# Expert attention with the turned probabilities as the moving operand, and two score passes on stacked queries, in a retention + MLP + expert-attention kernel

## The chip, the cores and the metric

The kernel runs as one program on one core of a Trainium2 chip. The metric is the device time in microseconds (us). The kernel before the change takes 551.65 us, the median of 3 runs (549.74 to 553.75). All durations below come from one profiled execution of it.

The core's engines work side by side and wait for each other through semaphores: TensorE (PE in the rows; PEld is its weight load), VectorE (DVE), ScalarE (ACT), GpSimd (POOL), and SyncE (SP), which here only issues DMAs.

## The reference, cut to what matters

```python
# 1. retention over q, k, v of (2, 8, 768, 64)           -> x (2, 768, 512)
# 2. x = x + relu(layernorm(x) @ w_ch1) @ w_ch2            (512 -> 2048 -> 512)
# 3. top-2 of 4 experts, each a causal attention of its own:
logits = x @ w_gate                          # (2, 768, 4)
w = softmax over the two largest logits
for e in range(4):
    q, k, v = x @ wq[e], x @ wk[e], x @ wv[e]          # (2, 768, 64) each
    scores = q @ k.T / 8, causal
    a = exp(scores - rowmax); a /= a.sum(-1) + 1e-9    # (2, 768, 768)
    ye = a @ v @ wo[e]                                 # (2, 768, 512)
    out += (w of this expert where it is chosen) * ye
```

All of it is float32. The change is in part 3 alone.

## The kernel before, in words

Every float32 product on TensorE is made of rounded parts: an operand is split into a high part (`hi`, rounded to the matmul format) and the rest (`lo`). ScalarE writes `hi` out of PSUM, VectorE subtracts and writes `lo`, and TensorE makes three passes, hi·hi, hi·lo and lo·hi (`PASSES`). Queries are tiled by 128 rows, six tiles for each of the two batches.

The program is an order written out by hand for each engine; semaphores only say when a step may start. Part 3 works on *units*: one unit is a query tile `i` of a batch `b` against its (i+1)·128 keys. `TILES = (5, 0, 4, 1, 3, 2)` puts a long and a short one together, so each *pair* of units has 7·128 = 896 score columns. One expert is 6 pairs, four experts are 24 pairs. A pair goes through these steps:

- `scores`: TensorE, 3 passes of q (stationary) against k (moving, up to 512 columns). q and k of the two batches lie on 64 rows each; the other batch's rows of k are zeros. A bf16 matmul adds the causal mask (`masked`).
- `row_max` on VectorE, `exponent` on ScalarE (exp with the sum of the row, `den`), `sum_plus`/`sum_inverse` on VectorE, `z_factor` on GpSimd (expert weight over the sum, one number a row).
- `turn_a`: TensorE transposes the 7 blocks of the pair into PSUM; `a_t_hi` (ScalarE) and `a_t_lo` (VectorE) write the two parts of the turned probabilities.
- `attend`: for each key block, `a_t` hi and lo are stationary and the 128 columns of `ev` (64 of v hi, 64 of v lo) are moved past them: 14 matmuls of 128 columns a pair.
- `z_lows` (ScalarE) and `z_add` (VectorE) scale and add the two halves of the result.

In four of the six pairs (`FILL`) TensorE also makes a quarter of the next expert's q and k (`expert_qk`, 12 matmuls of 384 columns), which `project_out` takes out of PSUM on ScalarE, `keys_lo` on VectorE and `queries_hi`/`queries_lo` per tile on both. In the last expert, `turn_z`, `z_t_hi`, `z_t_lo`, `output` and `output_out` follow each pair. Experts 0 to 2 are a hardware loop (`Fori`) on most engines, so each turn of it also spends register instructions on the counts to wait for.

In a pair, TensorE's order is `turn_a`, `scores` of the pair one ahead, `expert_qk`, `attend`.

Of the kernel before, what the change touches and what calls it, by code (L numbers as in the profile page):

```python
# [32 lines left out]
P = 128  # L33
# [36 lines left out]
def retention_moe_program(nc, q, k, v, g_ln, w_ch1, w_ch2, w_gate, wq, wk, wv, wo, out):  # L70
# [5 lines left out]
    NC = S // P  # L76
    KT = DM // P
# [5 lines left out]
    G = 3  # L83
    VG = E * D + E
# [12 lines left out]
    with ExitStack() as ctx:  # L97
# [6 lines left out]

        x = sb(ctx, "x", [P, NIT, NC, P])
# [19 lines left out]
        x2, w_o, eq_t = {}, {}, {}  # L125
# [46 lines left out]
        neg_max = sb(ctx, "neg_max", [P, 2])  # L172
        den = sb(ctx, "den", [P, B * NC])
        inv_den = sb(ctx, "inv_den", [P, B * NC])
        z_scale = sb(ctx, "z_scale", [P, B * NC])
        z_low = sb(ctx, "z_low", [P, 2, D])
        a = sb(ctx, "a", [P, 2, S])
        a_t = {part: sb(ctx, f"a_t_{part}", [P, 2, NC, P], F32R) for part in ("hi", "lo")}
        z = sb(ctx, "z", [P, B * NC, E * D])
        out_sb = sb(ctx, "out_sb", [P, 3, DM])  # L180
# [34 lines left out]
        s_pj, s_eqn, s_ekhi, s_eklo = (sem(n) for n in ("s_pj", "s_eqn", "s_ekhi", "s_eklo"))  # L215
        s_eqhi, s_eqlo, s_zero = sem("s_eqhi"), sem("s_eqlo"), sem("s_zero")
        s_sc, s_max, s_exp = sem("s_sc"), sem("s_max"), sem("s_exp")
        s_at, s_athi, s_atlo = sem("s_at"), sem("s_athi"), sem("s_atlo")
        s_pv, s_den, s_scl, s_zlow, s_z = (sem(n) for n in ("s_pv", "s_den", "s_scl", "s_zlow", "s_z"))
        s_wohi, s_wo, s_zt, s_zthi, s_ztlo = (sem(n) for n in ("s_wohi", "s_wo", "s_zt", "s_zthi", "s_ztlo"))  # L220
        s_out, s_osb = sem("s_out"), sem("s_osb")
# [35 lines left out]
        UNITS = [(TILES[2 * m_ + w], b) for m_ in range(3) for b in range(B) for w in range(2)]  # L257
        LAST_USE = {i: max(u for u, (i_, b) in enumerate(UNITS) if i_ == i) for i in TILES}
        NU = len(UNITS)
        PAIRS = NU // 2  # L260
        PJ = [(b, h) for b in range(B) for h in range(2)]
        HALF = S // 2


# [6 lines left out]
        def v_bank(t):  # L271


            return ps[:, t % 2 if t < EARLY else (6, 7, 3, 6)[t - EARLY], 0:VG]

        def ahead(e, p_):

            return (e, p_) if p_ < PAIRS else (e + 1, p_ - PAIRS)

# [3 lines left out]
        def sc_bank(u, a0, a1):  # L283

            return (flat(2, 3, a1) if u % 2 else flat(0, 2, a1))[:, a0:a1]

        def pj_bank(e, n):

            return ps[:, 2 + n if isinstance(e, int) and e == 0 else 3, 0:HALF]

        def at_bank(u, n):
            return flat(7, 8, n) if u % 2 else flat(4, 6, n)


# [1074 lines left out]
```

## Time and profile before

| | us |
|---|---|
| median of 3 runs | 551.65 |
| the profiled execution, its own time | 551.49 |
| its span, first to last instruction | 549.7 |
| TensorE busy | 526.0 (96%) |
| VectorE busy | 214.0 (39%) |
| ScalarE busy | 183.0 (33%) |
| GpSimd busy | 85.9 (16%) |
| granted clock, mean | 0.994 of full speed |
| retention | 0 to about 97 |
| MLP | about 97 to 374 |
| values, gate, q and k of expert 0 | 374 to 404 |
| four experts' attention | 404 to 549.7 |

The span is what lies between the first and last instruction; 1.8 us of the execution's time lie around it. The duration of a matmul in a row includes its pipeline, so neighbours overlap: how fast TensorE works is read from how far apart the starts lie, and the chain of waits gives a run of matmuls its length in that sense (12 matmuls of 512 columns in 2.80 us).

### The profile page before, as it was taken

How to read it: one execution, taken by the hardware profiler on the slowest of the kernel's cores; microseconds unless marked ns; L12 is line 12 of the kernel's file. 1: busy time of each engine (PE TensorE's matmuls, PEld its weight loads, DVE VectorE, ACT ScalarE, POOL GpSimd, SP SyncE). 2: the span in 40 equal slices, each digit the busy share in tenths (PEclk: the TensorE clock that was granted, in tenths of full speed). 3: DMA queues.
4: the chain of work that ended last, by engine and by line, in shares of the span. 5: the costliest groups of instructions: out<-in, count | busy, mean ns of one | idle time of the engine just before them, and what ended most of it. 6: DMA issues, size and time to landing. Idle time of an engine off the chain costs nothing.

```text
span 549.7 us, 8473 instructions
## 1 busy us (share of the span) xinstructions
PE 526.0 (96%) x3064; PEld 458.1 (83%) x3064; DVE 214.0 (39%) x519; ACT 183.0 (33%) x451; POOL 85.9 (16%) x113
## 2 busy tenths in 40 slices
PE   3999897999999999999999999999999999999997
PEld 2989897888888888888888888889989898988885
DVE  2444546313221422211141111235366565656562
ACT  3334341211010220101031101224466757667553
POOL 3000010899970000000000000005010100100000
PEclk9999998899999999999999999999999999999999
DMA  9474660344440000000000000000000000000123
GB/s 189 72 149 89 129 150 20 97 135 135 134 116 0 1 0 0 0 0 0 0 0 0 1 0 1 0 2 20 1 20 1 21 0 0 0 0 0 39 77 116
DMA packets 57948, 23.56 MB, mean 43 GB/s; under 512 B 45760, under 2 KB 54080, under 8 KB 57920
## 3 DMA queue, kind: packets, MB, share of 16 engines
q1 hardware_dynamic: 57920, 23.18, 17.7%
q8 instruction: 18, 0.29, 0.2%
q14 instruction: 10, 0.08, 0.0%
HBM read 20.03 MB, written 3.15 MB: 42 GB/s over the span
## 4 chain that ended last, share of the span: by engine, by line
PE 83%; DVE 7%; issue 5%; ACT 3%; POOL 1%; DVEq 0%; ACTq 0%; POOLq 0%
PE ps L567 24%; PE ps L576 24%; PE ps L667 5%; PE ps L711 4%; PE ps L684 4%; PE ps L487 3%; PE ps L643 3%; PE ps L734 3%; PE ps L508 3%; PE ps L696 2%; PE ps L500 2%; PE ps L513 2%; PE ps L475 2%; DVE neg_max L1263 1%; DVE scaled_k L252 1%
## 5 line engine op out<-in xcount | busy, mean ns | idle before, releaser
L1157 DVE SCALAR_TENSOR_TENSOR h_t_lo<-ps,h_t_hi 128x512 fp32r<-128x512 f32 x48 | 33.2, 691 | 200.0 <-ACT h_t_hi L843 200.0
L843 ACT ACTIVATE h_t_hi<-ps 128x512 fp32r<-128x512 f32 x48 | 28.7, 599 | 221.8 <-PE ps L567 221.8
L567 PE MATMUL ps<-xn_t_hi,w_hi 128*128 128x512 f32 x192 | 76.3, 397 | 0.9 <-DVE xn_t_lo L1152 0.9
L576 PE MATMUL ps<-w_hi,h_t_hi 128*128 128x512 f32 x192 | 76.1, 396 | 0.0
L567 PE MATMUL ps<-xn_t_lo,w_hi 128*128 128x512 f32 x192 | 75.9, 395 | 0.0
L567 PE MATMUL ps<-xn_t_hi,w_lo 128*128 128x512 f32 x192 | 75.7, 394 | 0.0
L576 PE MATMUL ps<-w_hi,h_t_lo 128*128 128x512 f32 x192 | 75.5, 393 | 0.0
L576 PE MATMUL ps<-w_lo,h_t_hi 128*128 128x512 f32 x192 | 74.6, 389 | 0.0
L567 PEld LDWEIGHTS ps<-xn_t_hi,w_hi 128*128 128x128 f32 x192 | 36.1, 188 | 9.3 <-issue 1.1
L567 PEld LDWEIGHTS ps<-xn_t_hi,w_lo 128*128 128x128 f32 x192 | 36.2, 189 | 8.6
L567 PEld LDWEIGHTS ps<-xn_t_lo,w_hi 128*128 128x128 f32 x192 | 36.3, 189 | 8.2
L576 PEld LDWEIGHTS ps<-w_hi,h_t_lo 128*128 128x128 f32 x192 | 36.0, 188 | 8.4
L576 PEld LDWEIGHTS ps<-w_lo,h_t_hi 128*128 128x128 f32 x192 | 36.1, 188 | 8.0
L576 PEld LDWEIGHTS ps<-w_hi,h_t_hi 128*128 128x128 f32 x192 | 36.0, 188 | 7.5
L937 ACT ACTIVATE a<-ps,neg_max 128x768 f32<-128x768 f32 (+5 forms) x48 | 30.0, 631 | 36.8 <-DVE neg_max L1263 36.8
L433 POOL TENSOR_TENSOR w_qk_lo<-raw_qk,w_qk_hi 128x512 fp32r<-128x512 f32 x4 | 5.1, 1280 | 229.3 <-ACT w_qk_hi L895 229.3
L711 PE MATMUL ps<-ev,a_t_hi 128*128 (+1 forms) x168 | 38.4, 272 | 0.7 <-DVE z_t_lo L1294 0.5
L711 PE MATMUL ps<-ev,a_t_lo 128*128 (+1 forms) x168 | 38.8, 275 | 0.0
L711 PEld LDWEIGHTS ps<-ev,a_t_hi 128*128 128x128 f32 x168 | 32.2, 191 | 1.9 <-DVE a_t_lo L1269 1.2
L1269 DVE TENSOR_TENSOR a_t_lo<-ps,a_t_hi 128x512 fp32r<-128x512 f32 (+2 forms) x64 | 30.1, 494 | 5.8 <-ACT a_t_hi L943 5.7
L711 PEld LDWEIGHTS ps<-ev,a_t_lo 128*128 128x128 f32 x168 | 32.2, 192 | 0.1
L487 PE MATMUL ps<-q_t,k_t 128*128 128x128 f32 x192 | 27.4, 289 | 1.6 <-ACT q_t L793 1.6
(136 smaller groups left out, 966.2 us busy)
## 6 DMA issues: line engine op xcount, KB each, us to landing
raw_w<-in_moe_w_ch SPq DMA_DIRECT2D x32, 256.0 KB, 2.6
raw_k<-in_k SPq DMA_DIRECT2D x16, 192.0 KB, 3.8
raw_q<-in_q SPq DMA_DIRECT2D x16, 192.0 KB, 4.3
raw_v<-in_v SPq DMA_DIRECT2D x16, 192.0 KB, 3.2
out_y<-out_sb SPq DMA_DIRECT2D x12, 256.0 KB, 2.0
raw_vg<-in_moe_wv SPq DMA_DIRECT2D x4, 128.0 KB, 2.9
raw_wo<-in_moe_wo SPq DMA_DIRECT2D x1, 512.0 KB, 4.7
raw_qk<-in_moe_wq SPq DMA_DIRECT2D x4, 128.0 KB, 2.1
```

The costliest lines, as they stand in the source:

```text
L487: mm = pe.matmul(s_bank(it, m_)[:, c, j], k_t[:, it % 2, 2 * m_ + c, j, :], q_t[:, it % 2, 2 * m_ + c, :], start=True, stop=True)
L508: mm = pe.matmul(y_bank(it, m_)[:, c % 2, j], prob[:, m_, c % 2, j, :], raw["v"][:, it % 2, c, j], start=(j == 0), stop=(c == 0), skip_gro ...
L567: mm = pe.matmul(ps[:, f % 2, :], w1[a_][:, f, kk, :], xn_t[b_][:, kk, :], start=(kk == 0 and p_ == 0), stop=(kk == KT - 1 and p_ == 2))
L576: mm = pe.matmul(ps[:, 2 + tau, :], h_t[a_][:, f % 2, tau * P:(tau + 1) * P], w2[b_][:, f, :], start=(f == 0 and p_ == 0), stop=(f == NF - ...
L643: mm = pe.matmul(v_bank(t), x2[a_][:, b, kk, c * P:(c + 1) * P], w_vg[b_][:, kk, :], start=(kk == 0 and p_ == 0), stop=(kk == KT - 1 and p ...
L667: mm = pe.matmul(pj_bank(e, n), w_qk[a_][:, kk, :], x2[b_][:, b, kk, half * HALF:(half + 1) * HALF], start=(kk == 0 and p_ == 0), stop=(kk ...
L684: mm = pe.matmul(sc_bank(u, a0, a1), eq_t[a_][:, i * P:(i + 1) * P], ek_t[b_][:, e % 2, b, a0:a1], start=(p_ == 0), stop=(p_ == 2 and not ...
L711: mm = pe.matmul(z_bank(u), a_t[a_][:, u % 2, sc, :], ev[:, b * NC + sc, e], start=(sc == 0 and a_ == "hi"), stop=(sc == i and a_ == "lo"))
L843: act.activation(h_t["hi"][:, f % 2, :], ps[:, f % 2, :], ACT.Relu).then_inc(s_hhi, 1)
L937: act.activation(a[:, u % 2, 0:n], sc_bank(u, 0, n), ACT.Exp, bias=neg_max[:, u % 2:u % 2 + 1], accum_out=den[:, u:u + 1]).then_inc(s_exp, 1)
L1157: dve.scalar_tensor_tensor(h_t["lo"][:, f % 2, :], ps[:, f % 2, :], 0.0, f32(h_t["hi"][:, f % 2, :]), ALU.max, ALU.subtract).then_inc(s_hl ...
L1269: dve.tensor_tensor(a_t["lo"][:, u % 2].rearrange("p c t -> p (c t)")[:, a0:a1], at_bank(u, a1)[:, a0:a1], f32(a_t["hi"][:, u % 2].rearran ...
```

## The change: what it does

1. **Attend.** The operands change sides: `ev` of a key block (128 columns: v hi and v lo) is stationary, and the turned probabilities are moved past it, three query tiles at a time (up to 384 columns, fewer at the diagonal). For that, `a_t` of three tiles is kept side by side (`a_top` for tiles 0 to 2, `a_low` for 3 to 5), and `attend(h)` runs once per *half* (expert and batch: 3 pairs), not once per pair: 18 matmuls for three pairs where there were 42. Units are now ordered by batch.
2. **z.** Its result comes out already turned, 128 rows by 384 columns, so `turn_z` and `z_t` from PSUM go. `z_lows`, `z_add` handle 64×384 tiles; new steps `z_round` (ScalarE) and `z_rest` (GpSimd) split z into hi and lo.
3. **Scaling.** A factor per row can no longer be applied after `attend`, so GpSimd's `weigh` multiplies the whole probabilities (896 columns a pair) before they are turned. Scores are now made two pairs ahead.
4. **Scores.** `q_both` holds q hi on rows 0 to 63 and q lo on rows 64 to 127; `k_twice` holds the same k on both. Two passes (k hi, k lo) give all four products. The second copy of k is a DMA from rows 64–127 to rows 0–63 (`repeat_k`, 8 an expert).
5. **Projection.** `project_lo` on VectorE now makes both k lo and q lo, 64×384 each; `queries_hi`/`queries_lo` and the zeroing of `ek_t` go.
6. **Start and end.** All `values` and the gate come before `expert_qk(0, ...)`; the hardware loops become plain repeated code; the outputs of batch 0 are made in the last two pairs, those of batch 1 after the last `attend`.

```diff
-        UNITS = [(TILES[2 * m_ + w], b) for m_ in range(3) for b in range(B) for w in range(2)]
+        UNITS = [(i, b) for b in range(B) for i in TILES]
-        FILL = (0, 1, 2, 4)
+        FILL = {1: 0, 2: 1, 4: 2, 5: 3}
...
+            def repeat_k(e, n):
+                b, half = PJ[n]
+                cols = slice(half * HALF, (half + 1) * HALF)
+                for part, s in (("hi", s_ekhi), ("lo", s_eklo)):
+                    sp.wait_ge(s, len(PJ) * e + n + 1)
+                    sp.dma_start(f32(k_twice[part][0:D, e % 2, b, cols]),
+                                 f32(k_twice[part][D:2 * D, e % 2, b, cols])).then_inc(s_twice[b], 16)
...
+            def weigh(g, w):
+                e, b, i, u, c0, c1 = span_of(g, w)
+                if w == 0:
+                    pool.wait_ge(s_den, 2 * g + 2)
...
+                pool.tensor_scalar(a[:, g % 2, c0:c1], a[:, g % 2, c0:c1], inv_den[:, u:u + 1],
+                                   weight[:, u, e:e + 1], ALU.mult, ALU.mult).then_inc(s_weighed, 1)
...
-                    for p_, (a_, b_) in enumerate(PASSES):
-                        mm = pe.matmul(sc_bank(u, a0, a1), eq_t[a_][:, i * P:(i + 1) * P],
-                                       ek_t[b_][:, e % 2, b, a0:a1], start=(p_ == 0), stop=(p_ == 2 and not diagonal))
+                        for part in ("hi", "lo"):
+                            mm = pe.matmul(sc_bank(g, a1)[:, a0:a1], q_both[:, e % 2, b, i * P:(i + 1) * P],
+                                           k_twice[part][:, e % 2, b, a0 - c0:a1 - c0],
+                                           start=(part == "hi"), stop=(part == "lo" and not diagonal))
...
-                for sc in range(i + 1):
-                    for a_ in ("hi", "lo"):
-                        mm = pe.matmul(z_bank(u), a_t[a_][:, u % 2, sc, :], ev[:, b * NC + sc, e],
-                                       start=(sc == 0 and a_ == "hi"), stop=(sc == i and a_ == "lo"))
+            def attend(h):
+                e, b = divmod(h, B)
+                for low in range(2):
+                    pe.wait_ge(s_atlo, at_count(G * (h + 1)))
+                    if h >= 1:
+                        pe.wait_ge(s_zsum, 2 * h - 1 + low)
+                    for s in (s_eqlo, s_eklo):
+                        pe.wait_ge(s, pieces_before(G * (h + 1)))
+                    last = G * (low + 1) - 1
+                    for sc in range(last + 1):
+                        skip = max(0, sc - G * low) * P
+                        for part in ("hi", "lo"):
+                            mm = pe.matmul(z_bank(low == 0)[:, skip:HALF],
+                                           ev[:, b * NC + sc, e].rearrange("p h d -> p (h d)"),
+                                           (a_low if low else a_top)[part][:, sc, skip:HALF], ...)
...
+            def slot(g):                                   # TensorE
+                e, p_ = divmod(g, PAIRS)
+                if g + 2 < LAST:
+                    scores(g + 2)
...
+                if g % G == 0 and g > 0:
+                    attend(g // G - 1)
+                turn_a(g)
+                if e < E - 1 and p_ in FILL:
+                    expert_qk(e + 1, FILL[p_], g)
...
+            def slot(g):                                   # VectorE
...
+                if g % G == 0:
+                    if g + 2 < LAST:
+                        for w in range(2):
+                            row_max(g + 2, w)
+                        sums(g + 2)
+                    if g > 0:
+                        for top in range(2):
+                            z_add(2 * (g // G) - 2 + top)
+                    for w in range(2):
+                        a_t_lo(g, w)
+                else:
+                    for w in range(2):
+                        if g + 2 < LAST:
+                            row_max(g + 2, w)
+                        a_t_lo(g, w)
+                    if g + 2 < LAST:
+                        sums(g + 2)
+                if e < E - 1 and p_ in FILL:
+                    project_lo(e + 1, FILL[p_])
```

How the order moves on VectorE, in a pair of the expert loop that has a fill piece. Names: `a_t_lo` and, in the change, `a_low_lo`, `a_top_lo` are the turned probabilities' low parts, `neg_max` the row maxima, `inv_den` the row sums, `ek_t_lo`/`k_twice_lo` the keys' low part. Before:

```order
L1278 TENSOR_SCALAR inv_den<-den 128x2 [waits s_exp]
L1268 REGISTER_ALU
L1269 TENSOR_TENSOR a_t_lo<-ps,a_t_hi 128x512 [waits s_athi]
L1268 REGISTER_ALU
L1269 TENSOR_TENSOR a_t_lo<-ps,a_t_hi 128x128 [waits s_athi]
L1282 ISA
L1283 RECIPROCAL inv_den<-inv_den 128x2 [waits s_den]
```

and with the change, the second pair of a half:

```order
L1290 TENSOR_REDUCE neg_max<-ps 128x1 [waits s_sc]
L1299 TENSOR_TENSOR a_low_lo<-ps,a_low_hi 128x4x128 [waits s_athi]
L1290 TENSOR_REDUCE neg_max<-ps 128x1 [waits s_sc]
L1299 TENSOR_TENSOR a_low_lo<-ps,a_low_hi 128x128 [waits s_athi]
L1299 TENSOR_TENSOR a_top_lo<-ps,a_top_hi 128x2x128
L1309 TENSOR_SCALAR inv_den<-den 128x2 [waits s_weighed,s_exp]
L1311 RECIPROCAL inv_den<-inv_den 128x2 [waits s_den]
L1280 TENSOR_TENSOR k_twice_lo<-ps,k_twice_hi 64x384 [waits s_ekhi]
L1283 SCALAR_TENSOR_TENSOR q_both<-ps,q_both 64x384 [waits s_eqhi]
```

The maxima now stand between the low parts, and the low part of q has joined that of k; register instructions are gone.

On ScalarE the same pair reads as follows with the change (`a,den<-ps,neg_max` is `exponent`, `k_twice_hi` and `q_both` are `project_out`):

```order
L975 ACTIVATE a_low_hi<-ps 128x4x128
L964 ACTIVATE a,den<-ps,neg_max 128x768
L975 ACTIVATE a_low_hi<-ps 128x128
L975 ACTIVATE a_top_hi<-ps 128x2x128
L964 ACTIVATE a,den<-ps,neg_max 128x128
L953 ACTIVATE k_twice_hi<-ps 64x384
L955 ACTIVATE q_both<-ps 64x384
```

The first `exponent` now stands between the two parts of `a_t_hi`; before, all of `a_t_hi` came first, in one run, and the exponents after it.

On TensorE, at the boundary between two halves (`k_twice` against `q_both` is `scores`, `a_top_hi,ev` is `attend`):

```order
L713 MATMUL ps<-x_hi,w_qk_lo 128x384
L731 MATMUL ps<-k_twice_hi,q_both 128x512 [waits s_exp,s_twice0,s_eqlo]
L731 MATMUL ps<-k_twice_lo,q_both 128x512
L735 MATMUL ps<-masked,ident_bf 128x128
L731 MATMUL ps<-k_twice_hi,q_both 128x384
L731 MATMUL ps<-k_twice_lo,q_both 128x384
L735 MATMUL ps<-masked,ident_bf 128x128
L762 MATMUL ps<-a_top_hi,ev 128x384 [waits s_eqlo,s_eklo,s_zsum,s_atlo]
```

`attend` waits for the low parts of the projection of the pair just before it (`s_eqlo`, `s_eklo`), since its PSUM banks are those that the projection used.

## Rows read from the trace of the kernel before

**Rows 1.** Page, the granted clock in 40 slices of the span, in tenths.
```profile
PEclk9999998899999999999999999999999999999999
```

**Rows 2.** Busy time by stretch (one expert): stretch, length, each engine's busy us (instructions), clock.
```profile
470.50:503.00 32.50, 32.34 (x234) 30.03 (x234) 20.33 (x62) 21.52 (x67) 1.16 (x6) 1.00 0.00 0
```

**Rows 3.** Chain of waits, one pair of expert 1: start us, us, what.
```profile
442.39 1.51 PE ps L711 x14
443.90 0.79 PE ps L696 x7
444.69 0.97 PE ps L684 x6
...
445.74 0.40 PE ps L684 x3
446.21 2.16 PE ps L667 x12
```

**Rows 4.** Chain of waits: values, projection of expert 0, gate's end, last expert, last eviction.
```profile
383.68 4.35 PE ps L643 x36
388.03 8.45 PE ps L667 x48
...
407.30 0.05 DVE weight L1243
...
519.95 1.42 PE ps L734 x6
...
522.13 0.44 PE ps L721 x4
...
546.66 0.60 ACT out_sb L965
```

**Rows 5.** Timeline, ScalarE and VectorE in that pair: start, us, instruction, [idle before <-releaser].
```profile
440.31 0.15 DVE L1283 RECIPROCAL inv_den<-inv_den 128x2 f32<-128x2 f32 x1
440.38 0.27 DVE L1269 TENSOR_TENSOR a_t_lo<-ps,a_t_hi 128x128 fp32r<-128x128 f32 x1
440.57 1.14 DVE L1263 TENSOR_REDUCE neg_max<-ps 128x1 f32<-128x768 f32 x2
441.55 0.90 ACT L937 ACTIVATE a<-ps,neg_max 128x768 f32<-128x768 f32 x1 [1.31 <-DVE neg_max L1263]
442.44 0.36 ACT L937 ACTIVATE a<-ps,neg_max 128x128 f32<-128x128 f32 x1
443.28 0.49 ACT L919 ACTIVATE ek_t_hi<-ps 64x384 f32 x1
443.99 0.56 DVE L1251 TENSOR_TENSOR ek_t_lo<-ps,ek_t_hi 64x384 f32 x1 [1.47 <-ACT ek_t_hi L919]
444.03 0.52 ACT L950 ACTIVATE z_low<-ps,z_scale 128x64 f32<-128x64 f32 x2 [0.26 <-PE ps L711]
444.44 1.04 ACT L943 ACTIVATE a_t_hi<-ps 128x512 fp32r<-128x512 f32 x3
```

**Rows 6.** Groups by line and shape, from 385 us on, VectorE and GpSimd.
```profile
L1269 DVE TENSOR_TENSOR a_t_lo<-ps,a_t_hi 128x512 fp32r<-128x512 f32 x24 | 16.5, 686 | 5.8 <-ACT a_t_hi L943 5.7
L1269 DVE TENSOR_TENSOR a_t_lo<-ps,a_t_hi 128x256 fp32r<-128x256 f32 x16 | 6.5, 408 | 0.0
L433 POOL TENSOR_TENSOR w_qk_lo<-raw_qk,w_qk_hi 128x512 fp32r<-128x512 f32 x3 | 3.8, 1281 | 14.3 <-ACT w_qk_hi L895 14.3
```

**Rows 7.** Groups by line and shape, whole span, GpSimd.
```profile
L409 POOL TENSOR_SCALAR w_hi<-raw_w 128x512 fp32r<-128x512 f32 x16 | 10.0, 623 | 74.2 <-DMA raw_w<-in_moe_w_ch 74.2
```

**Rows 8.** Page, a DMA: engine, count, KB each, median us from issue to landing.
```profile
raw_qk<-in_moe_wq SPq DMA_DIRECT2D x4, 128.0 KB, 2.1
```

**Rows 9.** Timeline of TensorE at the end of retention.
```profile
93.73 0.77 PE L500 MATMUL ps<-raw_v,scaled_k 128*128 128x128 f32 x2 [1.58 <-DVE state L1043]
```

**Rows 10.** Busy time by stretch, columns as in rows 2: the clock around it.
```profile
92.00:93.00 1.00, 0.15 (x2) 0.00 (x0) 0.96 (x4) 0.00 (x0) 0.00 (x0) 0.88 0.00 0
...
99.00:100.00 1.00, 1.00 (x7) 0.86 (x6) 0.00 (x0) 0.71 (x2) 1.00 (x2) 0.71 0.00 0
```

More of the change, by code:

```diff
@@ L102, in sem @@
             return ctx.enter_context(nc.semaphore(name))
+        with ExitStack() as late:
+            z_t = {part: sb(late, f"z_t_{part}", [P, 2, B, S], F32R) for part in ("hi", "lo")}
         x = sb(ctx, "x", [P, NIT, NC, P])
@@ L116, in retention_moe_program @@
             state = sb(early, "state", [P, NC - 1, P])
+        with ExitStack() as late:
+            z_low = sb(late, "z_low", [P, 2, HALF])
+            z_sum = sb(late, "z_sum", [P, 2, HALF])
         raw_vg = sb(ctx, "raw_vg", [P, KT, VG])
@@ L316, in norm_groups, with pj_bank, pieces_before, out_bank @@
+        FILL = {1: 0, 2: 1, 4: 2, 5: 3}
+        def pj_bank(n):
+            return ps[:, 6 + n % 2, 0:HALF]
+        def pieces_before(g):
+            return len(PJ) + sum(1 for g_ in range(g) if g_ < LAST - PAIRS and g_ % PAIRS in FILL)
+        def out_bank(o):
+            return ps[:, o % 2, :]
         def norm_groups(n):
@@ L462, in _ @@
+            for q in range(2 * HALVES - 2, 2 * HALVES):
+                z_rest(q)
         @block.tensor
@@ new lines, in expert_qk @@
+                if len(PJ) * e + n >= 2:
+                    pe.wait_ge(s_eqlo, len(PJ) * e + n - 1)
+                    pe.wait_ge(s_eklo, len(PJ) * e + n - 1)
+                if g >= G:
+                    pe.wait_ge(s_zsum, 2 * (g // G))
+                for kk in range(KT):
+                    for p_, (a_, b_) in enumerate(PASSES):
+                        mm = pe.matmul(pj_bank(n), w_qk[a_][:, kk, :], x2[b_][:, b, kk, half * HALF:(half + 1) * HALF],
+                                       start=(kk == 0 and p_ == 0), stop=(kk == KT - 1 and p_ == 2))
@@ new lines, in a_t_lo, with sums @@
+            def a_t_lo(g, bank):
+                dve.wait_ge(s_athi, at_count(g) + 1 if bank == 0 else at_count(g + 1))
+                for part in at_parts(g):
+                    if part[0] == bank:
+                        dve.tensor_tensor(a_t("lo", part), at_source(g, part), f32(a_t("hi", part)),
+                                          ALU.subtract).then_inc(s_atlo, 1)
+            def sums(g):
+                u = span_of(g, 0)[3]
+                pair = slice(u, u + 2)
+                dve.wait_ge(s_exp, 2 * g + 2)
+                if g >= PAIRS:
+                    dve.wait_ge(s_weighed, 2 * (g - PAIRS) + 2)
@@ L1346, in _ @@
             gate_out()
-            with dve.Fori(0, E - 1) as e:
-                expert(e, False)
-            expert(E - 1, True)
-            z_t_lo(PAIRS - 1)
+            for n in range(3):
+                project_lo(0, n)
+            for w in range(2):
+                row_max(0, w)
+            sums(0)
+            project_lo(0, 3)
+            for w in range(2):
+                row_max(1, w)
+            sums(1)
+            for g in range(LAST):
+                slot(g)
+            for q in range(2 * HALVES - 2, 2 * HALVES):
+                z_add(q)
+            for o in range(NC + 1, 2 * NC, 2):
+                output_out(o)
 _INS = ["q", "k", "v", "moe_g_ln", "moe_w_ch1", "moe_w_ch2", "moe2_w_gate", "moe2_wq", "moe2_wk", "moe2_wv", "moe2_wo"]
```

549 lines of the change are left out of this document (250 added, 299 removed).

## The prediction, made before the changed kernel ran

> **What bounds the kernel now.** I read the clock first: it is full nearly everywhere, also in all of the attention stage [rows 1]. Then the busy time by stretch. One expert takes 32.5 us, and in it TensorE is busy for 32.34, ScalarE 21.5, VectorE 20.3, GpSimd 1.2 [rows 2]. Then the chain of waits inside a pair: it runs through TensorE alone, 1.51 attend, 0.79 transposes, 0.97 + 0.40 scores (the masks add 0.07 each), 2.16 projection, together 5.97 us [rows 3]. So in the middle of an expert TensorE sets the pace. But the timeline of the same pair shows how near the next bound is: ScalarE waits only 0.26 us for `attend` before `z_low` [rows 5]. ScalarE and VectorE hand work to each other and back, in strict order, and that ring is nearly as long as TensorE's list. That is the point on which this prediction turns.
>
> **TensorE: what goes.** Attend: 14 matmuls of 128 columns in 1.51 us is 0.108 each [rows 3], 336 of them 36.2 us. By widths, 384 columns take 0.18 (12 in 2.16 [rows 3]), 260 take 0.121 (36 in 4.35 [rows 4]), 128 take 0.108. A half now has ten of 384, four of 256, four of 128: 1.80 + 0.48 + 0.43 = 2.7 us, eight halves 21.7. Saved: 14.5. Scores: the third of three passes, (0.97 + 0.40)/3 = 0.46 a pair, 24 pairs: 11.0. `turn_z`: 0.44 a pair, six: 2.6 [rows 4]. Together 28 us less TensorE work. A half (three pairs) then needs scores 3 × 1.05, transposes 3 × 0.79, projection 2 × 2.16, attend 2.7: 12.6 us, where it took 16.3.
>
> **The ring of ScalarE and VectorE: what stays.** I walk VectorE's list for one half, since it is the engine that is waited for. On VectorE the next instruction starts 0.08 before the last one's end (0.27 at 440.38, next at 440.57 [rows 5]), so I take duration less 0.08; on ScalarE three `a_t_hi` take 1.04, so the second part costs 0.55 after the first. Handing over costs about 0.04: the first maximum took 0.94 and the exponent began 0.98 after it began [rows 5]. In the first three experts register instructions still lie in such gaps; the change has none.
>
> - Second pair: max 768 0.87; `a_t_lo` 512 0.61 [rows 6]; max 128 0.28 (with its end, as the exponent needs both); 0.04; exponent 768 0.89 to the next start [rows 5]; `a_t_hi` 128+256 0.55, which stands behind that exponent in ScalarE's queue; 0.05; `a_t_lo` 128+256 0.19+0.33 [rows 5, 6]; the two small sum operations 0.30 (0.15 each [rows 5], one waits for the other); k lo and q lo 0.48 each (0.56 [rows 5]; the second operation I take like the first). Sum 5.1.
> - Third pair: the same with 640/256 and 384 in place of 768/128 and 128+256: 4.9 (the long max and exponent are 0.1 shorter each).
> - First pair: maxima 1.15, both exponents 1.35 with the last one's accumulator, sums 0.30, two `z_add` of 64×384 0.96, `a_t_lo` 1.13, hand-overs and short waits for `z_low` and `a_t_hi` 0.3. Sum 5.2.
>
> A half is 15.2. TensorE's part in it: `attend` can't start before the last q lo, as its banks are the projection's, and `z_low` of its second part and the transposes behind it then arrive 0.1 late. So 15.3 us a half, where TensorE needs 12.6 and stands still for 2.7, in one piece, ahead of `attend`. Check of the method on before: the ring of a pair with projection gives 5.4 to 5.7 against TensorE's 5.97, and the 0.26 wait agrees. So each half gains 1.0 us, not 3.7: the rest of the saving becomes a wait.
>
> GpSimd hides: `weigh` of 896 columns costs 1.1 to 1.3 by 0.62 for 512 [rows 7], `z_rest` 1.0 by 1.28 for 512 [rows 6]; 7 us of `weigh` an expert beside 30.6, and scores are two pairs ahead, so nobody waits. If that cover went, each pair would pay 1.3. The DMA copies of k (about 2.1 us to land [rows 8]) are needed more than 3 us after they are issued, except at the start.
>
> **The start.** Values now end at 388.03 + 4 × 1.45 = 393.8 [rows 4]. The gate's chain ends 3.9 later: in before the last values ended at about 388.03 + 8.45 projection + 5.8 values + 1.5 scores of a pair = 403.8 and the gate at 407.35 [rows 3, 4], 3.6 later, and I add 0.3, since no other work lies between the gate's steps now. From there, one behind the other: k lo and q lo of two pieces (to +6.0), the copy of k (+7.8), scores (+8.9), maxima and exponents of the first pair (+11.6), fourth projection piece on both engines (+13.1), the same for the second pair (+15.9). So the first pair's ring begins at 409.7, some 5 us later than in before. What was filled with values before is a wait now.
>
> **Sum.** 409.7, first half without z 14.2, then 423.9; five halves of 15.3: 500.4; one half without projection, 15.3 − 1.9 = 13.4: 513.8. End: z of the last but one half is split 5.95 later, then TensorE is dense: six outputs of 1.42 [rows 4] and two transposes, 10.2, `attend` 2.7; the turned z goes through four engines' steps (0.5 + 0.5 + 0.5 + 1.0, the first part hidden behind `attend`'s second), 1.1 more; six outputs 8.6; eviction and last DMA 3.2 (549.7 − 546.66 in before [rows 4], and 0.2 for the pipeline's end). That is 31.8 and an end at 545.6. Around the span lie 1.8 us: 547.4.
>
> **The clock.** At the end of retention TensorE stood still for 1.58 us after sparse work [rows 9], and the clock fell to half, from within the slice at 92 until within the slice at 99 [rows 10]. The change adds a stand-still of 2.7 us in each half. Work around it is denser than it was there, so I don't expect a fall each time. What one costs: while the clock is at 1.2 GHz, `attend` and the transposes behind it, 3.5 us, take up to twice as long, and in the first pair of a half VectorE waits for them. I price a fall at 1.7 (partly beside `attend`) to 3.0 (all of `attend` and some transposes) and put two of them at 1.7 into the number: 547.4 + 3.4 = **551 us**, against the profiled 551.5 and the median 551.65. No change that can be measured: I take 1%, 5.5 us, as what a measurement tells.
>
> The Trainium skill (TensorE: Matmul & The Clock Gate, "Why this matters for your kernels") advises against idle gaps of TensorE of a length that a gap of 2.7 us does not reach. By that rule no fall would come, and the time would be 547.4; the trace before speaks against it, with a fall after 1.58 us.
>
> **Rivals.**
>
> A. *Slower: the clock falls in nearly each half.* Seven stand-stills at 3.0 each are 21: 547.4 + 21 = 568. It decides from 9.5 us of falls in all on (above 557), three to five of them. For it: the fall in rows 9 and 10 after a shorter stop, and that the stop sits right ahead of the work on which VectorE waits. Against: the full clock through retention [rows 1], where TensorE also waits in each iteration, though shorter. Chance 0.22.
>
> B. *The ring is shorter than I walk it.* If ScalarE and VectorE overlap more (no register instructions, hand-overs of nearly nothing), a half might be 14.3; 6.9 halves give 7 less and fewer stops: 541. Against: each term is a measured duration. Chance 0.15.
>
> C. *TensorE keeps the pace, as the change hopes.* Then 551.5 − 28 + 5 at the start = 528. It needs VectorE's list to run without the waits for ScalarE (1.5 us in each pair, as the 1.47 in rows 5), which the order forbids. Chance 0.07.
>
> D. *My forecast*: the ring sets the pace, with none to three falls, 547 to 556. Chance 0.56.
>
> **Numbers.** Faster by over 1% (below 546.1): B, C and a little of D, 0.26. Slower by over 1% (above 557.2): A and a little of D, 0.24. Within: 0.50. The range leaves out C and the worst of A: 539 to 565. Unknown in D itself: the start (±2) and 0.2 in each pair's ring (±4).
>
> **What would show it.** In the profile after: an expert of 30 to 31 us; VectorE and ScalarE each busy for 20 to 21 of it; the chain of waits in the loop going through VectorE and ScalarE and not TensorE; TensorE waiting before `attend` for `q_both` of the piece before; the second part of `a_t_lo` waiting for ScalarE in each pair. Attend's matmuls at 0.18 apart and 144 of them; score matmuls 128. The clock below full in some stretches behind those waits would show the price of the stop. Wrong would be: TensorE without waits in the loop (then C), or waits on GpSimd's `a` or on the copies of k, which I hold for hidden.

## The result: 580.2 us, 5% slower, and outside the range

The changed kernel takes 580.2 us (median of 4 runs, 579.5 to 581.1) against 552.0 (549.7 to 553.8) for the kernel before on the same chip: ratio 1.051 [1.047, 1.056]. Forecast were 551, with a range to 565. The profiled execution has a span of 577.7 us, where the sum without clock falls gave 545.6.

First the page of the changed kernel: the granted clock, and the copies of k.

```profile
PEclk9999997999999999999999999999798779997789
k_twice_hi<-k_twice_hi SPq DMA_DIRECT2D x16, 96.0 KB, 2.1
```

Where [rows 1] show a full clock, there are now gaps from slice 29 on (each is 14.4 us; slice 29 begins at 404 us). The copies land in 2.1 us, as assumed, and in the loop no engine's list of waits names them.

Then the busy time by stretch, columns as in [rows 2]: stretch, length, busy us (instructions) of TensorE, its weight load, VectorE, ScalarE and GpSimd, then the clock, the DMA share and GB/s. A stretch is one half (three pairs), cut where VectorE starts the two maxima of the half's first pair. The first half has no `attend`, five have everything, the seventh has no projection, and the last stretch is the last half with the end.

```profile
405.00:421.25 16.25, 11.49 (x60) 10.55 (x59) 10.21 (x25) 9.12 (x25) 6.69 (x9) 0.79 0.12 29
421.25:439.80 18.55, 12.81 (x85) 11.79 (x85) 11.11 (x26) 11.10 (x29) 6.27 (x9) 1.00 0.09 22
439.80:461.58 21.78, 17.00 (x85) 16.04 (x85) 11.11 (x26) 10.70 (x28) 7.54 (x10) 0.76 0.13 31
461.58:482.52 20.94, 15.92 (x85) 14.90 (x85) 11.12 (x26) 11.34 (x29) 6.27 (x9) 0.84 0.08 19
482.52:501.28 18.76, 12.82 (x85) 11.80 (x85) 11.13 (x26) 10.71 (x28) 7.53 (x10) 1.00 0.09 22
501.28:521.56 20.28, 14.37 (x85) 13.36 (x85) 11.11 (x26) 10.59 (x28) 6.29 (x9) 0.92 0.08 21
521.56:539.59 18.03, 13.03 (x62) 11.52 (x63) 8.69 (x22) 8.75 (x24) 5.06 (x7) 0.72 0.04 10
539.59:577.70 38.11, 28.41 (x129) 24.02 (x129) 11.34 (x23) 11.86 (x26) 6.84 (x8) 0.87 0.22 83
```

Two things are to be read here. In the two halves at full clock TensorE is busy for 12.8 us, as the 12.6 of the forecast, so its work did go down. But those halves take 18.55 and 18.76 us, 18.65 on average, where 15.3 were forecast, and no engine is busy for more than 13 of them. The five halves that have everything take 20.06 us on average; what is over 18.65 goes with the clock, which is below full in the other three.

What fills the 18.55 is in the timeline of the first such half (TensorE, ScalarE, VectorE; most rows left out).

```profile
421.25 1.16 DVE L1290 TENSOR_REDUCE neg_max<-ps 128x1 f32<-128x512 f32 x2
421.32 0.41 PE L762 MATMUL ps<-a_top_hi,ev 128*128 128x384 f32 x1 [2.09 <-DVE q_both L1283]
...
424.01 0.95 PE L746 MATMUL ps<-ident,a 128*128 128x128 f32 x7
...
425.06 0.69 ACT L964 ACTIVATE a<-ps,neg_max 128x512 f32<-128x512 f32 x1 [4.51 <-PE ps L746]
...
426.44 0.17 DVE L1309 TENSOR_SCALAR inv_den<-den 128x2 f32<-128x2 f32 x1 [4.03 <-ACT a L964]
...
428.79 1.05 PE L746 MATMUL ps<-ident,a 128*128 128x128 f32 x7 [2.75 <-DVE a_low_lo L1299]
...
429.09 0.95 DVE L1290 TENSOR_REDUCE neg_max<-ps 128x1 f32<-128x768 f32 x1
...
432.47 0.29 DVE L1299 TENSOR_TENSOR a_low_lo<-ps,a_low_hi 128x128 fp32r<-128x128 f32 x1 [1.50 <-ACT a_top_hi L975]
...
434.57 0.82 DVE L1290 TENSOR_REDUCE neg_max<-ps 128x1 f32<-128x640 f32 x1
...
437.66 0.56 DVE L1299 TENSOR_TENSOR a_top_lo<-ps,a_top_hi 128x384 fp32r<-128x384 f32 x1 [1.33 <-ACT a_top_hi L975]
...
439.80 1.16 DVE L1290 TENSOR_REDUCE neg_max<-ps 128x1 f32<-128x512 f32 x2
```

`L1290` are the maxima, `L762` is `attend`, `L746` the transposes (`turn_a`), `L964` the exponents, `L1309` the first of the two sum steps, `L1299` the low parts. The maxima are ready 1.2 us after 421.25, but the exponents start at 425.06, behind the transposes (L746). `exponent(g + 2)` writes the buffer `a[:, g % 2]` that `turn_a(g)` reads, and so waits for `s_at` (lines 961 to 963); and in the first pair of a half `turn_a(g)` stands on TensorE behind the 2.7 us of `attend`, which itself waits for VectorE's last `q_both`. So the ring, in which VectorE and ScalarE hand work to each other, is closed by a detour over TensorE. VectorE stands still for 4.0 us, and TensorE stands still twice: 2.09 ahead of `attend`, 2.75 ahead of the transposes of the second pair. The list of waits of the changed kernel sums it up (who <- for whom: us, times, longest):

```profile
DVE inv_den L1309 <- ACT a L964: 40.8, 10, 5.7
ACT a L964 <- PE ps L746: 38.5, 7, 6.2
...
PE ps L746 <- DVE a_low_lo L1299: 19.3, 7, 2.8
...
PE ps L762 <- DVE q_both L1283: 15.8, 6, 3.2
```

The forecast had also named waits on GpSimd's `a` as a sign of being wrong. The list has one, TensorE's weight load for the transposes, 17.2 us in 6 times. But GpSimd had finished the product of that pair at 421.46 (the last one begins at 420.90 and takes 0.56), 7 us before these transposes start; the low parts named above are what they waited for last. In the loop GpSimd is hidden, as forecast.

The second loss is the clock. In the timeline of TensorE, the two stops of the next half:

```profile
440.03 0.41 PE L762 MATMUL ps<-a_top_hi,ev 128*128 128x384 f32 x1 [3.15 <-DVE q_both L1283]
449.05 1.73 PE L746 MATMUL ps<-ident,a 128*128 128x128 f32 x7 [2.75 <-DVE a_low_lo L1299]
```

And the busy time of three stretches around them, columns as above:

```profile
442.00:444.00 2.00, 2.00 (x10) 2.00 (x9) 0.00 (x0) 0.00 (x0) 0.00 (x0) 0.50 0.57 130
...
446.00:448.00 2.00, 0.30 (x4) 0.17 (x2) 1.12 (x4) 1.95 (x7) 0.82 (x2) 1.00 0.00 0
...
450.00:452.00 2.00, 2.00 (x9) 2.00 (x8) 1.19 (x3) 0.87 (x2) 1.22 (x2) 0.50 0.00 0
```

At each of the two stops the clock goes to 0.50, that is 1.2 GHz. The first fall comes after the stop, when `attend` has run for about 1.2 us (1.00 until 441.20, 0.61 from there to 441.60, then 0.50); the second comes within the stop (1.00 until 448.00, 0.50 from 448.30 on). `attend`, for which both other engines wait, takes 4.1 us from its first start to its last end, where it took 2.9 in the half before.

### The profile page after: what moved, and what is told of

Its sections match the earlier page's. It is cut to its first block, busy times and chain, and to the rows that moved or that the text cites. A ratio compares the mean times of both kernels' runs of the same rounds, so it can differ in the third digit from the quotient of the medians.

```text
span 577.7 us, 7555 instructions
## 1 busy us (share of the span) xinstructions
PE 509.9 (88%) x2784; PEld 447.6 (77%) x2784; DVE 218.8 (38%) x475; ACT 178.5 (31%) x403; POOL 126.3 (22%) x151
## 3 DMA queue, kind: packets, MB, share of 16 engines
HBM read 20.03 MB, written 3.15 MB: 40 GB/s over the span
## 4 chain that ended last, share of the span: by engine, by line
PE 76%; DVE 11%; ACT 6%; issue 5%; POOL 1%; ACTq 0%; DVEq 0%; POOLq 0%
PE ps L610 23%; PE ps L619 23%; PE ps L762 5%; PE ps L530 3%; PE ps L780 3%; PE ps L713 3%; PE ps L686 3%; PE ps L746 3%; PE ps L551 2%; ACT a L964 2%; DVE a_low_lo L1299 2%; PE ps L543 2%; DVE neg_max L1290 2%; PE ps L556 2%; PE ps L518 2%
## 5 line engine op out<-in xcount | busy, mean ns | idle before, releaser
L610 PE MATMUL ps<-xn_t_hi,w_hi 128*128 128x512 f32 x192 | 74.9, 390 | 0.8 <-DVE xn_t_lo L1182 0.8
L610 PE MATMUL ps<-xn_t_lo,w_hi 128*128 128x512 f32 x192 | 74.7, 389 | 0.0
L473 POOL TENSOR_SCALAR a<-a,inv_den,weight 128x768 f32<-128x768 f32 (+5 forms) x48 | 34.0, 719 | 117.6 <-DVE inv_den L1311 117.6
L964 ACT ACTIVATE a<-ps,neg_max 128x768 f32<-128x768 f32 (+5 forms) x48 | 30.4, 634 | 61.7 <-PE ps L746 38.5
L746 PE MATMUL ps<-ident,a 128*128 128x128 f32 x168 | 28.3, 317 | 19.7 <-DVE a_low_lo L1299 19.3
L746 PEld LDWEIGHTS ps<-ident,a 128*128 128x128 f32 x168 | 22.3, 165 | 21.8 <-POOL a L473 17.2
L1290 DVE TENSOR_REDUCE neg_max<-ps 128x1 f32<-128x768 f32 (+5 forms) x48 | 28.8, 617 | 0.5
L1299 DVE TENSOR_TENSOR a_low_lo<-ps,a_low_hi 128x512 fp32r<-128x512 f32 (+2 forms) x40 | 21.4, 554 | 18.0 <-ACT a_top_hi L975 10.5
```

The costliest lines, as they stand in the source:

```text
L473: pool.tensor_scalar(a[:, g % 2, c0:c1], a[:, g % 2, c0:c1], inv_den[:, u:u + 1], weight[:, u, e:e + 1], ALU.mult, ALU.mult).then_inc(s_we ...
L610: mm = pe.matmul(ps[:, f % 2, :], w1[a_][:, f, kk, :], xn_t[b_][:, kk, :], start=(kk == 0 and p_ == 0), stop=(kk == KT - 1 and p_ == 2))
L746: mm = pe.transpose(flat(4, 6, s0 + P)[:, s0:s0 + P], a[:, g % 2, s0:s0 + P], ident[:, :])
L964: act.activation(a[:, g % 2, c0:c1], sc_bank(g, c1)[:, c0:c1], ACT.Exp, bias=neg_max[:, 2 * (g % 2) + w:2 * (g % 2) + w + 1], accum_out=de ...
L1290: top = dve.tensor_reduce(neg_max[:, 2 * (g % 2) + w:2 * (g % 2) + w + 1], sc_bank(g, c1)[:, c0:c1], AX.X, ALU.max, negate=True)
L1299: dve.tensor_tensor(a_t("lo", part), at_source(g, part), f32(a_t("hi", part)), ALU.subtract).then_inc(s_atlo, 1)
```

## The experiments

All times are medians, ratios against the kernel before of the same session (551.0, 551.6, 552.0 and 552.3 us).

**The transposes ahead of attend.** On TensorE, in the first pair of a half:

```diff
+                turn_a(g)
                 if g % G == 0 and g > 0:
                     attend(g // G - 1)
-                turn_a(g)
```

> The changed kernel, with turn_a ahead of attend in the first pair of each half on TensorE (two lines swapped), nothing else. Theory 1, the missed wait: exponent of the pair two ahead overwrites the buffer that turn_a reads, so it waits for turn_a, and turn_a stands behind attend; VectorE then sits for 5.7 us in each half. Swapped, the exponents run beside attend, and a half at full clock goes from 18.6 to about 16.3 us: seven halves give 14 to 17 less, 563 to 566 us, and VectorE's 5.7 us waits for the exponents go. Theory 2, the clock: the halves are long because TensorE runs at 1.2 GHz in them; the swap only moves where it stands still, and the time stays within 5 us of 580.

Measured: 556.9 us, ratio 1.010 [1.006, 1.013]: 23 less, more than expected. Its first half at full clock and its first half below it:

```profile
421.88:437.82 15.94, 13.03 (x85) 11.70 (x85) 11.12 (x26) 11.12 (x29) 6.25 (x9) 1.00 0.11 26
437.82:455.50 17.68, 14.62 (x85) 13.30 (x85) 11.21 (x26) 10.68 (x28) 7.50 (x10) 0.90 0.16 38
```

A stretch of 2 us inside the second:

```profile
440.00:442.00 2.00, 2.00 (x9) 2.00 (x8) 0.89 (x3) 0.84 (x3) 1.14 (x2) 0.50 0.58 131
```

Its group of the first step of the row sums, which waits for both exponents (busy us, mean ns | idle before it, releaser):

```profile
L1309 DVE TENSOR_SCALAR inv_den<-den 128x2 f32<-128x2 f32 x24 | 4.1, 169 | 14.1 <-ACT a L964 14.1
```

In its first half at full clock, that step of the sums and the first maximum of the second pair:

```profile
424.44 0.17 DVE L1309 TENSOR_SCALAR inv_den<-den 128x2 f32<-128x2 f32 x1 [1.41 <-ACT a L964]
...
427.11 0.95 DVE L1290 TENSOR_REDUCE neg_max<-ps 128x1 f32<-128x768 f32 x1
```

A half at full clock takes 15.94 for 18.55, and VectorE waits 1.41 us for 4.03: the missed wait cost 2.6 us a half. What VectorE waits for exponents falls from 40.8 to 14.1 us. The clock still falls, in three of the five halves, which take 17.5 to 17.7.

**Other work in the stops.** Small bf16 matmuls, whose result nobody reads, in the two stops, 18 and 24 of them:

```diff
+            def keep_busy(g, n):
+                pe.wait_ge(s_exp, 2 * g + 4)
+                for _ in range(n):
+                    pe.matmul(sc_bank(g + 1, P)[:, :], ident_bf[:, :], masked[:, :], start=True, stop=True,
...
+                if g % G == 0 and G <= g < LAST - G:
+                    keep_busy(g, 18)
+                if g % G == 1 and G < g < LAST - G:
+                    keep_busy(g, 24)
```

> The changed kernel with filler matmuls (bf16, 128 columns, into a score bank that is free then) in TensorE's two stops of a half: 18 ahead of attend, 24 ahead of the transposes of the second pair. They take 1 to 2.7 us of stops of 2 to 4 us and compute nothing that is used. Theory 1 (missed wait): only what the half clock costs goes, 20.1 to 18.6 us a half, six halves and less at the end: 568 to 572 us. Theory 2 (clock first): the granted clock of the attention stage goes from about 0.85 to nearly 1, and with it the time from 580 to about 557, since 47 us at 1.2 GHz cost up to 23.

Measured: 574.4 us, ratio 1.040 [1.033, 1.048]: 6 less. That is above theory 1's 572, with single executions from 570.3 to 577.9, and far from theory 2's 557. Two of its halves:

```profile
442.03:460.75 18.72, 15.48 (x127) 14.11 (x127) 11.11 (x27) 10.58 (x28) 7.54 (x10) 1.00 0.15 36
460.75:481.07 20.32, 17.07 (x127) 15.71 (x127) 11.13 (x27) 11.23 (x29) 6.27 (x9) 0.92 0.09 21
```

Four of the five halves now run at full clock and take 18.5 to 18.8; the fifth is the second row. This parts the two losses: five times (20.06 - 18.65) is 7 us of clock, and 18.65 instead of 15.3 has nothing to do with it.

**The order in ScalarE's and VectorE's lists.** In the second and third pair both parts of `a_t_hi` ahead of both exponents, and both maxima ahead of both low parts (ScalarE's side; VectorE's is alike):

```diff
                     for w in range(2):
                         a_t_hi(g, w)
-                        if g + 2 < LAST:
+                    if g + 2 < LAST:
+                        for w in range(2):
                             exponent(g + 2, w)
```

> The changed kernel with ScalarE's order in the second and third pair of a half made a_t_hi, a_t_hi, exponent, exponent, and VectorE's row_max, row_max, a_t_lo, a_t_lo. Nothing is removed. If the ring of ScalarE and VectorE is what sets these pairs (as the prediction had it), VectorE no longer waits 1.3 to 1.5 us for the part behind the exponent, a pair with projection goes from 5.1 to about 4.1 us, 15 pairs: 565 to 570 us. If TensorE or its clock sets them, within 3 us of 580.

Measured: 565.2 us, ratio 1.027 [1.020, 1.035]: 15 less, as expected. Its two halves at full clock take 16.8 and 16.9, so the order is worth 1.8 of the 2.8 us (1.50 and 1.33) that VectorE waited inside the two pairs.

**Both together**, the two edits above in one kernel.

> Both edits, the swap of turn_a and attend and the two queues' order. If each removes its own wait in series, the savings add: 548 to 553 us, about the kernel before. If both only shift the same stop, about as the better one alone, 563 to 568.

Measured: 539.0 us, ratio 0.978 [0.974, 0.982], faster than before and by more than expected: the five halves take 14.1 to 14.3, and the clock is full in all of them. The two edits bring 38 us as the sum of the single runs and 41 together. I had expected 548 to 553 by adding what I expected of each; the swap alone had brought 23 rather than 14 to 17, and that the clock would be full in all five halves once both waits are gone I had not counted.

**A third buffer for the probabilities.** If the buffer is the reason, another buffer must do what the other order does:

```diff
-        a = sb(ctx, "a", [P, 2, WIDE])
+        a = sb(ctx, "a", [P, 3, WIDE])
...
-                if w == 0 and g >= 2:
+                if w == 0 and g >= 3:
 
-                    act.wait_ge(s_at, 2 * g - 2)
-                act.activation(a[:, g % 2, c0:c1], sc_bank(g, c1)[:, c0:c1], ACT.Exp,
+                    act.wait_ge(s_at, 2 * g - 4)
+                act.activation(a[:, g % 3, c0:c1], sc_bank(g, c1)[:, c0:c1], ACT.Exp,
```

> The changed kernel with a third buffer for a: exponent(g+2) then waits for the transposes of pair g-1, not of g, and TensorE's order stays as it is. Theory 1 (VectorE stands still for 5.7 us in each half because the exponents of the first pair overwrite the buffer that turn_a, behind attend, still reads): that wait goes, a half comes to about 15.5 to 16.5 us, and the time to 553 to 562. Rival 1 (what was wrong in the earlier swap's favour was the order on TensorE, attend ahead of the transposes, and not the buffer): the half stays at about 20 us and the time over 572. Rival 2 (the gain is the clock's alone): the time falls by what falls of the clock bring, 6 us or less.

Measured: 561.3 us, ratio 1.018 [1.012, 1.024]. TensorE's order is unchanged, and its half at full clock takes 15.97, the same as with the transposes first (15.94 and 16.10); VectorE's wait for the exponents is the same 14.1 us as well:

```profile
419.76:435.73 15.97, 12.81 (x85) 11.79 (x85) 11.12 (x26) 11.13 (x29) 6.27 (x9) 1.00 0.11 26
```

So it is the wait for the buffer, and the order only lengthened it. That the time is 4.4 us above the swap's goes with the clock: here four of the five halves are below full, there three.

**TensorE's saving given back.** One score pass more:

```diff
-                        for part in ("hi", "lo"):
+                        for n, part in enumerate(("hi", "lo", "lo")):
```

> The changed kernel with one score pass more (the pass with k's low part is done twice, so that small correction counts double in the values): 24 x 0.46 = 11 us of TensorE work come back. Theory 1 (in the changed kernel TensorE's work in the loop lies beside a longer ring of ScalarE and VectorE): the time moves by less than 4 us, either way, 576 to 584. Rival (TensorE's list is on the path, and the ring isn't): 11 us more, 588 to 592.

Measured: 575.8 us, ratio 1.044 [1.041, 1.047], 4.4 *less* than the changed kernel, a shade more than the 4 that theory 1 allowed, and the wrong way for the rival. A half at full clock:

```profile
420.33:438.89 18.56, 14.13 (x93) 12.98 (x93) 11.11 (x27) 11.22 (x29) 6.29 (x9) 1.00 0.09 22
```

TensorE works 1.3 us more (0.44 a pair, 0.46 in the forecast), the half takes 18.56 as before, and the stops are shorter: 1.4 to 2.3 us ahead of `attend` where they were 2.0 to 3.2, and 2.3 for 2.8 ahead of the second pair's transposes. The clock is higher, 0.976 over the span for 0.953, and with that the time goes down. TensorE's work is off the path here.

**The projection one pair earlier**, on top of both edits: `FILL = {0: 0, 1: 1, 3: 2, 4: 3}`.

> As the fourth kernel (transposes ahead of attend, parts of a_t_hi ahead of the exponents), and the four projection pieces of an expert one pair earlier (pairs 0, 1, 3, 4 of six in place of 1, 2, 4, 5), so that attend no longer stands right behind the last piece whose banks it takes. Theory 1 (attend's wait for the last q_both costs the half some tenths of a us there): 0 to 1 us less a half, 533 to 540. Rival (the piece behind attend now waits for z_add, which takes the same banks back, and VectorE gets a piece more into the pair that has z_add already): 0.5 to 1.5 us a half more, 542 to 550.

Measured: 544.5 us, ratio 0.987 [0.985, 0.989], 5.5 worse than without: halves of 15.4 to 15.6. The rival held: the projection behind `attend` (L713) now waits for `z_add`, and VectorE behind it for k's high part.

```profile
425.54 0.41 PE L713 MATMUL ps<-x_hi,w_qk_hi 128*128 128x384 f32 x1 [1.57 <-DVE z_sum L1320]
428.41 0.56 DVE L1281 TENSOR_TENSOR k_twice_lo<-ps,k_twice_hi 64x384 fp32r<-64x384 f32 x1 [1.81 <-ACT k_twice_hi L953]
```

**The last two slots.** On top of both edits, `turn_a(g)` ahead of `output(0)`, `output(2)` and `output(3)`, the evictions behind accordingly.

> As the fourth kernel, and in the last two slots the transposes stand ahead of the outputs on TensorE, with their evictions moved behind accordingly. In the fourth kernel's trace TensorE waits 3.7 us there for the turned z. Theory 1 (the end of the kernel is 38 us where 32 were forecast because the last slots' exponent, transposes and attend wait behind outputs that wait for z): 2 to 4 us less, 535 to 537. Rival (outputs only change places, and the last attend and the turning of z set the end): within 1 us of the fourth kernel, 538 to 540.

Measured: 535.6 us, ratio 0.972 [0.969, 0.974], 3.4 less than without. This is the fastest version. Four of its stretches, the last but one without projection, the last the end:

```profile
432.97:447.20 14.23, 12.84 (x85) 11.72 (x85) 11.12 (x27) 10.69 (x28) 7.50 (x10) 1.00 0.20 48
...
475.74:489.95 14.21, 12.82 (x85) 11.70 (x85) 11.12 (x26) 10.70 (x28) 6.26 (x9) 1.00 0.12 29
489.95:501.13 11.18, 9.17 (x62) 7.88 (x63) 8.70 (x22) 8.67 (x24) 5.04 (x7) 1.00 0.07 17
501.13:532.50 31.37, 24.34 (x123) 20.18 (x121) 11.34 (x23) 11.81 (x26) 6.84 (x8) 0.99 0.26 101
```

**Both remedies for the buffer at once**, the eighth kernel with the third buffer:

> The eighth kernel (transposes first, both parts of a_t_hi ahead of both exponents, the two last slots' outputs behind the transposes), and a third buffer for a besides. Theory 1 (with the transposes first, the exponents no longer wait for the buffer to speak of, so its two remedies don't add up): within 2 us of the eighth kernel, 533.5 to 537.5. Rival (the exponents of the first pair still wait for transposes for a good part of the time, one us or more in a half): 6 us or more less, below 530.

Measured: 535.8 us, ratio 0.971 [0.969, 0.973]: no difference: with the transposes first, a third buffer brings nothing more.

**The saving given back in the mended kernel**, the eighth with the pass of the sixth:

> The eighth kernel with one score pass more, as in the sixth (k's low part counts double): 11 us of TensorE work come back, where a half is 14.3 us and TensorE's list 12.6 plus 1.4. Theory 1 (also with the ring mended, ScalarE and VectorE set the pace, TensorE nearly does): 1 to 6 us more, 537 to 541. Rival (with the ring mended, TensorE's list is the pace): 8 to 12 us more, 543.5 to 548.

Measured: 537.8 us, ratio 0.975 [0.973, 0.977], 2.2 more for 11 us of work:

```profile
434.36:448.71 14.35, 13.91 (x96) 12.86 (x95) 11.11 (x26) 10.64 (x28) 7.49 (x10) 1.00 0.20 47
```

At 13.9 of 14.35 TensorE is now nearly the pace as well.

**Where the MLP's arrays lie.** The changed kernel began its values 4.9 us earlier (369.56 for 374.50, not the 4.5 of the expectation below), though nothing ahead of them was meant to change. The chain of waits of the kernel before in the MLP (start, us, what):

```profile
109.53 2.80 PE ps L567 x12
112.33 2.76 PE ps L576 x12
```

The same of the changed kernel:

```profile
109.61 2.72 PE ps L610 x12
112.33 2.72 PE ps L619 x12
```

The change makes `a_top` larger than what lay there, so the MLP's arrays behind it (`w2`, `h_t`, `xn_t`) move by 896 bytes. Two kernels differ from others in nothing but padding: the kernel before with 896 bytes more, and the eighth with 128 more, which makes the shift 1024 bytes:

```diff
+        sb(ctx, "rest", [P, 224])
```

and

```diff
-        sb(ctx, "rest_of_a_top", [P, 2 * G * G * P - 2 * KT * VG])
+        sb(ctx, "rest_of_a_top", [P, 2 * G * G * P - 2 * KT * VG + 32])
```

> The kernel before with one unused array of 224 floats (896 bytes) a partition behind w_vg, so that the MLP's arrays (w2, h_t, xn_t) lie where the change has put them; nothing else differs. In the changed kernel the MLP's matmuls of 512 columns come 2.72 us a dozen where they took 2.76 to 2.80 before, and the values begin 4.5 us earlier. Theory 1 (that gain comes from where the arrays lie, not from the attention code): the MLP goes at 2.72 a dozen here too, and the kernel takes 4 to 5 us less, 546 to 548. Rival (it comes from something else in the changed program): 550.5 to 552.5.

Measured: 546.7 us, ratio 0.989 [0.987, 0.992], 2.72 to 2.74 a dozen throughout.

> The eighth kernel with 32 floats (128 bytes) more of padding ahead of the MLP's arrays, which puts them back into the position modulo 1024 bytes that they have in the kernel before. Theory 1 (the position decides): the MLP goes back to 2.76 to 2.80 us a dozen, 4 to 5 us more than the eighth kernel, 539.5 to 541. Rival (it is something else): 534.5 to 536.5.

Measured: 541.3 us, ratio 0.981 [0.979, 0.984], 5.7 more than the eighth, and the old pattern in its chain of waits:

```profile
108.17 2.80 PE ps L610 x12
110.97 2.76 PE ps L619 x12
```

Both as theory 1 says, with 5.6 and 5.7 us even a little more than expected. In the traces the MLP, from its first 24 matmuls of 512 columns to the values, takes 268.5 us in the changed and the eighth kernel and 273.7 in the kernel before and the padded eighth, 5.1 more. Groups by line and shape, from 110 to 370 us, show which matmuls it is; the kernel before:

```profile
L567 PE MATMUL ps<-xn_t_hi,w_hi 128*128 128x512 f32 x183 | 72.6, 397 | 0.0
L576 PE MATMUL ps<-w_hi,h_t_hi 128*128 128x512 f32 x182 | 72.2, 397 | 0.0
L576 PE MATMUL ps<-w_lo,h_t_hi 128*128 128x512 f32 x182 | 70.7, 389 | 0.0
```

The kernel before with padding:

```profile
L577 PE MATMUL ps<-w_hi,h_t_hi 128*128 128x512 f32 x188 | 73.7, 392 | 0.0
L577 PE MATMUL ps<-w_lo,h_t_hi 128*128 128x512 f32 x189 | 73.6, 389 | 0.0
L568 PE MATMUL ps<-xn_t_hi,w_hi 128*128 128x512 f32 x184 | 71.8, 390 | 0.0
```

Some forms take 397 ns in one place and 390 to 392 in the other, one 389 in both. In the products with `xn_t` (L567, L568) only the moving operand has moved; in those with `h_t` (L576, L577) both operands have. Which of the arrays matters, and why, these runs don't tell.

## Why the prediction was wrong

The sum without falls gave 545.6, the span is 577.7. The 32.1 us between them, term by term. For the five halves, 18.65 is the mean of the two at full clock (18.55, 18.76), and 16.02 that of the first experiment's two (15.94, 16.10): 18.65 - 16.02 is the missed wait, 16.02 - 15.3 the size of the ring's other terms, 20.06 - 18.65 the clock.

| term | forecast | measured | difference |
|---|---|---|---|
| first maxima (start) | 409.7 | 405.0 | -4.7 |
| first half | 14.2 | 16.25 | +2.05 |
| five halves: missed wait | none | 5 x 2.63 | +13.2 |
| five halves: size of the ring | 15.3 | 16.02 | +3.6 |
| five halves: clock | none | 5 x 1.41 | +7.0 |
| half without projection | 13.4 | 18.03 | +4.6 |
| end | 31.8 | 38.1 | +6.3 |

**The step that failed** is the first pair of the ring: "maxima 1.15, both exponents 1.35 ..., Sum 5.2". It took the exponents to start as soon as the maxima are there, and left out what ScalarE waits for besides, the buffer that `turn_a` frees behind `attend`. Measured, the first pair takes 7.84 (421.25 to 429.09). With the transposes first it takes 5.23 (421.88 to 427.11), so the rest of that sum held: maxima 1.18 to the exponents' start, exponents 1.38, sums 0.51 with the hand-over, two `z_add` 1.03, low parts 1.13. The same wait is in the last two rows of the table: the swap alone takes the half without projection from 18.03 to 14.97 and the end from 38.1 to 33.7. The first half has no `attend` and not this wait. Of its 2.05 the order of the two lists is 0.95 (15.30 in the fourth kernel, at about the same clock, 0.78); the rest goes with that clock, but no run parts it.

**The clock** was right in kind and in the price of a fall, and too low in their number. I counted on one stop of 2.7 us a half; the missed wait made it two, of 2.0 to 3.2 and 2.75 to 2.8. I had priced a fall at 1.7 to 3.0 and put in two; three of the five halves ran below full clock, and they took 3.1, 2.3 and 1.6 more than 18.65. Rival A (falls in nearly each half, seven at 3.0) got the number of falls nearer than I did; at 1.4 a half on average, seven halves give 9.9, and 547.4 + 9.9 = 557 is not its 568. The Trainium skill (TensorE: Matmul & The Clock Gate, "Why this matters for your kernels"), by which no fall would come at a gap of 2.7 us, is not borne out: the row at 450 shows 0.50 after a stop of 2.75 us, within which the clock fell. The row at 442 doesn't speak on this, as its stop of 3.15 us is longer than the 2.7 for which the forecast cited that section; the first experiment does, with a fall after stops of 1.04 and 1.14.

**The ring's other two pairs** were forecast at 5.1 and 4.9 and took 5.48 and 5.23. k lo and q lo cost 0.58 to 0.59 each rather than 0.48 (433.40, 433.99, 434.57 in the trace), the two small sum operations 0.39 and 0.49 rather than 0.30, and the long maximum of the second pair 0.99 rather than 0.87, since the low part behind it waits for ScalarE's high part until 430.05. I had taken 0.08 off every duration for the overlap with the next instruction. Between k lo, q lo and the next maximum there is no overlap but 0.03 us of pause, while the maximum of 0.82 at 434.57 is followed at 435.32, with the overlap. What decides between the two isn't shown. The two waits inside a pair, 1.50 and 1.33, are of the length forecast (1.53 in the sum for the second pair); the 1.47 in [rows 5] was another wait, for the keys' high part.

**The claim that carried the forecast** held: TensorE's work left the path. It went from 16.2 (half of the 32.34 in [rows 2]) to 12.8 a half and the time did not follow; the sixth kernel gives 11 us of it back at no cost. Rival C is thereby excluded, for this order of the lists. With both orders changed a half is as short as rival B's 14.3, but by another mechanism than B's: the waits go, not the hand-overs.

**The end** was forecast at 31.8, took 38.1, and takes 31.4 in the eighth kernel. The missed wait with the slow clock (`attend` at 4.44) is 4.4 of the 6.3, by the swap's 33.7; outputs that stand ahead of the transposes while the turned z is not there are 2.4 (33.8 in the fourth kernel's trace, 31.4 in the eighth's). **The start**: from the end of the last values (388.9) to the first maxima 16.1 us, 15.9 forecast. The -4.7 is the MLP's, behind which the values began 4.9 us earlier for the place of its arrays, which I had not looked at. That is luck, and it made the miss look smaller than it was.

So the change has a gain that is not the attention's: by the padding in the kernel before and in the eighth, 5 to 6 us come from the arrays' place. Against the kernel before with its arrays in the same place (546.7) the changed kernel is 6% slower, and the fastest version (535.6) about 2% faster (2.0% by the medians, 1.8% by the two ratios); that is what the attention itself, mended, is worth here.

## What to carry to other kernels

When one engine is relieved, walk the ring of the others with every semaphore that each instruction waits for, those that free a buffer above all, and follow each to where its releaser stands in its own queue. A double buffer that sufficed while the engine behind it was the pace can become the longest wait once it isn't, and a producer's write can be freed by putting the reader ahead of longer work, at no cost. When a change moves an array, look at stages that it doesn't touch before crediting it with their time.

## What was unexpected of the hardware

Some matmuls of 512 columns took 397 ns each with their operands in one place and 390 to 392 with them 896 bytes elsewhere, 2.80 and 2.76 or 2.72 us a dozen, in two kernels both ways: 5 to 6 us in 550. And the clock did not answer to the length of one stop alone. In the changed kernel it stayed full through stops of 2.09 and 2.75 us (ending at 421.32 and 428.79), and fell after one of 3.15 and within one of 2.75 (ending at 440.03 and 449.05). In the first experiment it fell about a microsecond after two stops of only 1.04 and 1.14 us (ending at 436.39 and 438.05; 0.89 from 438.5 to 439.0, then 0.50). In the eighth kernel it stayed full over five halves in which 0.90 was the longest (418 to 490).
